# Two second layers at a time as seven products of halves, with the split input weights kept in device memory

## The chip, the cores and the metric

The kernel runs on one core of a Trainium2 chip. The metric is device time in microseconds (us) of one execution. TensorE (PE) multiplies, VectorE (DVE), ScalarE (ACT) and GpSimd (POOL) work on elements, and SyncE (SP) issues the DMAs.

## The reference, cut to what matters

```python
def reference(**kw):
    attn_out = _attn_ref(q, k, v)          # window of +-3 keys, and a branch pooled by 4; 4 x 8 heads x 576 x 64
    x = attn_out.transpose(0, 2, 1, 3).reshape(2304, 512)
    x = (sigmoid(x @ w_gate) * (x @ w_val)) @ w_out          # layer 1, 1536 hidden
    h = x @ w_in
    return (h * sigmoid(1.702 * h)) @ w_out2                 # layer 2, 2048 hidden
```

## The kernel before, in words

Attention is worked in 16 units (two heads of a batch each) and leaves x, transposed, in `att`: 512 features as 4 tiles of 128 partitions, 2304 tokens as three passes of 768. Both layers keep each pass in `att`: a layer's output takes the place of its input.

**Groups and phases.** A phase is one layer on one pass. Its hidden features are worked in groups of 256: 6 groups in layer 1 and 8 in layer 2, 42 in all, numbered k. The phases are (layer, pass) = (1,0), (1,1), (2,0), (1,2), (2,1), (2,2).

**Precision.** Every operand of a large product is a sum of a rounded part (hi) and a rest (lo), and a product is made as hi·hi + hi·lo + lo·hi. ScalarE rounds (`CAST`), GpSimd subtracts to get the lo part of weights and of x, VectorE that of the gated values g.

**Input products.** The product of x with a block of 256 hidden features is made by seven products of halves (p1 to p7, Winograd's form) of 6 matmuls of 128x384 each. A group has two blocks in layer 1 (gate and value), one in layer 2. GpSimd makes the four sums of weights that it needs, ScalarE and GpSimd split them, in each of the three phases of a layer anew from the weights as loaded (`w_raw`). VectorE combines the products (`c11`, `c12`, `c22`), ScalarE takes copies between them (`snap`), makes the gate (`sigmoid`/`gelu`) and rounds (`round_g`, L874). Three pairs of PSUM banks hold the quarters: `s_ps`, `d_ps`, `t_ps`.

**Second layer.** `second` multiplies g of a group by 256 rows of the output weights (`v_raw`, split as v_hi, v_lo) in the ordinary way through `passes` (L432): in layer 1 in 8 tiles of 6 matmuls of 384 columns, in layer 2 in 6 tiles of 6 matmuls of 512 columns. The tiles go by turns to the two banks of `o_ps`, and VectorE adds each to `att` (L1271). So TensorE's tile n waits until the tile n-2 has been added.

**Order.** Each engine's work is written out by hand, one list per engine, and an engine works its list strictly in turn; semaphores hold it where an operand isn't there. TensorE's list puts the second layer of group k between the input products of group k+1. SP's list holds the loads, each behind a wait for the buffer that it overwrites.

## Time and profile before

| | |
|---|---|
| median of 3 runs | 897.64 us (897.04 to 898.20) |
| the profiled execution: time, span | 896.92 us, 895.2 us |
| granted TensorE clock, mean | 1.00 |
| TensorE, VectorE, ScalarE, GpSimd busy | 99%, 53%, 54%, 78% |
| traffic of device memory, mean | 89 GB/s |

The span is the time between the first and the last instruction in the profile. An engine's busy time counts its operations, not its waits, and the chain that ended last says which engine's work and which waits the span is made of.

### The profile page before, as it was taken

What the parts mean: (1) busy time and instruction counts of PE and PEld (TensorE: products, weight loads), DVE (VectorE), ACT (ScalarE), POOL (GpSimd) and SP (SyncE); (2) the same over time, 40 slices, a digit from 0 to 9 for tenths busy, and PEclk for the clock granted to TensorE, in tenths of its full rate; (3) what the DMA queues carried; (4) which work ended last, traced back from release to release, by engine and by line L of the source; (5) the groups of instructions that cost most, each with busy time, mean ns of one, the idle gap of its engine ahead of it and who ended that gap; (6) DMA issues with size and microseconds to landing.
All of it is one profiled execution on the core that took longest, in us unless ns stands there. A gap on an engine that the chain in (4) does not pass through costs nothing.

```text
span 895.2 us, 17338 instructions
## 1 busy us (share of the span) xinstructions
PE 887.3 (99%) x6572; PEld 831.2 (93%) x6572; DVE 472.2 (53%) x865; ACT 483.5 (54%) x967; POOL 694.8 (78%) x551
## 2 busy tenths in 40 slices
PE   8999999999999999999999999999999999999998
PEld 6878899999999999999898899999998999989897
DVE  5767545555555455554544455555545445454545
ACT  5777755554445455545555455544645554545542
POOL 6679989998779999758787869998757887566551
PEclk9999999999999999999999999999999999999999
DMA  9776112222221222222221222422222212132111
GB/s 333 251 226 219 54 62 71 71 69 74 69 67 55 71 72 71 71 71 71 71 71 52 67 72 70 141 72 71 71 72 68 74 48 93 50 120 92 48 48 70
DMA packets 26722, 80.38 MB, mean 90 GB/s; under 512 B 2960, under 2 KB 3216, under 8 KB 26640
## 3 DMA queue, kind: packets, MB, share of 16 engines
q1 hardware_dynamic: 26640, 79.28, 27.5%
q8 instruction: 52, 0.85, 0.4%
q14 instruction: 30, 0.25, 0.1%
HBM read 74.55 MB, written 4.72 MB: 89 GB/s over the span
## 4 chain that ended last, share of the span: by engine, by line
PE 98%; DMA 1%; SPq 1%; issue 0%; DVE 0%
PE o_ps L432 39%; PE d_ps L442 7%; PE d_ps L445 7%; PE d_ps L444 7%; PE s_ps L442 6%; PE s_ps L445 6%; PE s_ps L444 6%; PE t_ps L442 3%; PE t_ps L445 3%; PE t_ps L444 3%; PE o_ps L405 1%; PE o_ps L425 1%; PE t_ps L376 1%; PE t_ps L417 1%; PE s_ps L330 1%; PE t_ps L390 1%
## 5 line engine op out<-in xcount | busy, mean ns | idle before, releaser
L1271 DVE TENSOR_TENSOR att<-o_ps,att 128x512 f32<-128x512 f32 (+1 forms) x245 | 152.4, 626 | 150.5 <-PE o_ps L432 150.5
L1518 POOL TENSOR_TENSOR w_lo<-w_sum,w_hi 128x1024 fp32r<-128x1024 f32 x60 | 144.1, 2402 | 66.0 <-ACT w_hi L782 66.0
L1513 POOL TENSOR_TENSOR w_lo<-w_raw,w_hi 128x768 fp32r<-128x768 f32 x60 | 111.0, 1849 | 44.1 <-ACT w_hi L778 44.1
L442 PE MATMUL d_ps<-xs_hi,w_hi 128*128 128x384 f32 x360 | 120.5, 335 | 0.0
L445 PE MATMUL d_ps<-xs_hi,w_lo 128*128 128x384 f32 x360 | 120.4, 335 | 0.0
L444 PE MATMUL d_ps<-xs_lo,w_hi 128*128 128x384 f32 x360 | 120.4, 334 | 0.0
L1531 POOL TENSOR_TENSOR v_lo<-v_raw,v_hi 128x1024 fp32r<-128x1024 f32 x42 | 100.7, 2398 | 20.3 <-ACT v_hi L786 20.3
L432 PE MATMUL o_ps<-v_hi,g_hi 128*128 128x512 f32 x288 | 111.9, 389 | 0.8 <-DVE att L1271 0.8
L432 PE MATMUL o_ps<-v_hi,g_lo 128*128 128x512 f32 x288 | 112.3, 390 | 0.0
L432 PE MATMUL o_ps<-v_lo,g_hi 128*128 128x512 f32 x288 | 112.3, 390 | 0.0
L1492 POOL TENSOR_TENSOR w_sum<-w_raw 128x256 f32<-128x256 f32 x120 | 88.4, 736 | 23.6 <-PE t_ps L445 20.2
L442 PE MATMUL s_ps<-xs_hi,w_hi 128*128 128x384 f32 x300 | 100.8, 336 | 0.0
L445 PE MATMUL s_ps<-xs_hi,w_lo 128*128 128x384 f32 x300 | 100.4, 335 | 0.0
L444 PE MATMUL s_ps<-xs_lo,w_hi 128*128 128x384 f32 x300 | 100.4, 335 | 0.0
L432 PE MATMUL o_ps<-g_hi,v_hi 128*128 128x384 f32 x288 | 96.3, 335 | 0.0
L432 PE MATMUL o_ps<-g_hi,v_lo 128*128 128x384 f32 x288 | 96.2, 334 | 0.0
L432 PE MATMUL o_ps<-g_lo,v_hi 128*128 128x384 f32 x288 | 96.2, 334 | 0.0
L782 ACT CAST w_hi<-w_sum 128x1024 fp32r<-128x1024 f32 x60 | 63.3, 1055 | 20.6 <-POOL w_sum L1492 20.4
L1215 DVE TENSOR_TENSOR g_lo<-t_ps,g_hi 128x384 fp32r<-128x384 f32 x90 | 49.8, 553 | 45.6 <-ACT g_hi L874 45.6
L442 PEld LDWEIGHTS d_ps<-xs_hi,w_hi 128*128 128x128 f32 x360 | 67.6, 188 | 0.6
L444 PEld LDWEIGHTS d_ps<-xs_lo,w_hi 128*128 128x128 f32 x360 | 67.6, 188 | 0.5
L445 PEld LDWEIGHTS d_ps<-xs_hi,w_lo 128*128 128x128 f32 x360 | 67.6, 188 | 0.0
(135 smaller groups left out, 1993.6 us busy)
## 6 DMA issues: line engine op xcount, KB each, us to landing
v_raw<-in_w_out_dram SPq DMA_DIRECT2D x42, 512.0 KB, 3.5
w_raw<-in_w_gate_val_dram SPq DMA_DIRECT2D x36, 512.0 KB, 3.6
w_raw<-in_w_in_dram SPq DMA_DIRECT2D x24, 512.0 KB, 3.5
vw<-in_v_win_dram SPq DMA_DIRECT2D x16, 390.0 KB, 4.9
vt<-in_v_tok_dram SPq DMA_DIRECT2D x16, 320.0 KB, 3.8
qk<-in_q_t_dram SPq DMA_DIRECT2D x16, 288.0 KB, 3.5
qk<-in_k_t_dram SPq DMA_DIRECT2D x16, 288.0 KB, 4.5
out_dram<-att SPq DMA_DIRECT2D x17, 256.0 KB, 4.5
```

What stands on the lines that cost most here:

```text
L330: mm = pe.matmul(s_ps[HK * par:HK * par + QW, h, pair * KW:(pair + 1) * KW], qu[rows, 0, PAD + at:PAD + at + QW], qu[rows, 1, at:at + KW], ...
L432: mm = pe.matmul(bank, a, b, start=(i == 0), stop=(i == len(steps) - 1))
L442: pe.matmul(bank, wh[:, w, cols], xh[:, x, c, :], start=(start and c == 0), stop=False, skip_group_check=True)
L444: pe.matmul(bank, wh[:, w, cols], xl[:, x, c, :], start=False, stop=False, skip_group_check=True)
L445: mm = pe.matmul(bank, wl[:, w, cols], xh[:, x, c, :], start=False, stop=(c == 1), skip_group_check=True)
L782: nc.scalar.copy(w_hi[b % 2][:, S1:S4 + 1, :], w_sum[b % 2][:, S1:S4 + 1, :]).then_inc(wshi_ready, 1)
L1215: vec.tensor_tensor(g_lo[k % 2][:, t, f, :], bank[LAST[k] % 2], g_hi[k % 2][:, t, f, :], ALU.subtract).then_inc(g_ready[n], 1)
L1271: vec.tensor_tensor(part, value, part, ALU.add).then_inc(y_added, 1)
L1492: return gp.tensor_tensor(w_sum[b % 2][:, name, :], a, c, op)
L1513: gp.tensor_tensor(w_lo[b % 2][:, A11:A22 + 1, :], w_raw[b % 2][:, R11:R22 + 1, :], w_hi[b % 2][:, A11:A22 + 1, :], ALU.subtract).then_inc ...
L1518: gp.tensor_tensor(w_lo[b % 2][:, S1:S4 + 1, :], w_sum[b % 2][:, S1:S4 + 1, :], w_hi[b % 2][:, S1:S4 + 1, :], ALU.subtract).then_inc(ws_re ...
L1531: gp.tensor_tensor(v_lo[k % 2][:, :, :], v_raw[k % 2][:, :, :], v_hi[k % 2][:, :, :], ALU.subtract).then_inc(v_ready, 1)
```

## The change

From the second phase on, groups go in pairs (c, d = c+1), and n = c+2 is the next pair's first. Phase 0 (groups 0 to 5) stays as it was.

1. **Second layers.** `second_pair` makes the second layers of c and d together as seven products of halves (`TILES`), two tiles each: 14 tiles of 6 matmuls of 384 columns for a pair. Its right operands are g's quarters and four sums of them, T1 to T4, which VectorE makes in PSUM (`make_t1` ...) and splits (`low_t1` ...) and ScalarE rounds (`hi_t1` ...), with copies of quarters by ScalarE (`save11`, `save12`, `save21`). Its left operands are seven pieces of the output weights of both groups (two loads into `raw`): ScalarE rounds them (`v_a12`, `v_s1`, `v_a11`, `v_s2`, `v_s4`, `v_s3`, `v_a22`), GpSimd makes four sums and seven lo parts (`split_pair`), 11 operations of 128x2x256 a pair. All 14 tiles of a pair come after the first five input products of n; p4 and p3 of n follow the tiles.
2. **Input weights.** In phase 0 the split weights of layer 1 are written to device memory (`w_split`), and those of layer 2 are split in eight separate `job`s between the pairs of phases 0 to 2 (ScalarE: `job_a`, `job_s`; GpSimd: `job_sums`, `job_lows`) and written there too. All later blocks fetch them (`fetch_12`: 786 KB and 525 KB, `fetch_3`: twice 262 KB a block); ScalarE and GpSimd don't split input weights there any more.
3. **x.** The seven split quarters and sums of x lie in a ring of 10 in place of two sets of seven. So those of the next phase are in part made early (`early_x`), and in part only when the phase's last block has read the place (`late_x`, `wait_last`), ahead of `split_pair` of the next phase's first pair in GpSimd's list.
4. **Phases** are (1,0), (1,1), (1,2), (2,0), (2,1), (2,2). The output is stored a pass at a time, the last one by tiles.

```diff
+RING = 10
...
-PHASES = [(1, 0), (1, 1), (2, 0), (1, 2), (2, 1), (2, 2)]
+OB1 = 2 * KC
+PHASES = [(1, 0), (1, 1), (1, 2), (2, 0), (2, 1), (2, 2)]
...
+TILES = ((VA12, B21, True, 0, 0), (VS1, T1, True, 1, 1), (VS4, B22, False, 0, 1), (VA11, B11, True, 0, 0),
+         (VS2, T2, False, 0, 1), (VS3, T3, False, 1, 1), (VA22, T4, False, 1, 0))
+OBP = 2 * NP
+SINCE = (8, 6, 10, 6, 4, 8, 14)
+G_OUT = {g: 2 * i + 2 for i, (v, g, start, r, t) in enumerate(TILES)}
+V_OUT = {v: 2 * i + 2 for i, (v, g, start, r, t) in enumerate(TILES)}
...
+def ring(q, x):
+    return (NP * q + x) % RING
...
+        w_split = nc.dram_tensor("w_split", (MADE + JOBS, P, 2, NP, WG), F32).ap()
...
+            def fetch_12(b):
+                if b >= NB:
+                    return
+                if b < MADE + 2:
+                    sp.wait_ge(spilled[b % 2], 16 * (MADE // 2))
+                if b == FIRST[NL1]:
+                    sp.wait_ge(job_stored, 16 * JOBS)
+                sp.wait_ge(in_done[b % 2], count(b - 2, 3))
+                sp.dma_start(w[b % 2][:, :, A11:S2 + 1, :].bitcast(F32), w_split[split_at(b), :, :, A11:S2 + 1, :]).then_inc(w_in1[b % 2], 16)
+                sp.wait_ge(in_done[b % 2], count(b - 2, 5))
+                sp.dma_start(w[b % 2][:, :, S1:S3 + 1, :].bitcast(F32), w_split[split_at(b), :, :, S1:S3 + 1, :]).then_inc(w_in2s[b % 2], 16)
...
+            def load_pair(c):
+                if c >= NG:
+                    return
+                if c == G1:
+                    sp.wait_ge(wa_ready, MADE)
+                    sp.wait_ge(wsum_ready, MADE)
+                else:
+                    sp.wait_ge(vp_ready, NP * pair(c))
+                q, lay, p, g = GROUPS[c]
+                source = w_out1 if lay == 1 else w_out2
+                for i in range(2):
+                    sp.dma_start(raw[:, i, :, :].rearrange("p a n -> p (a n)"), source[g + i]).then_inc(vp_loaded, 16)
...
+            def second_pair(c, i):
+                v_part, g_part, start, r, t = TILES[i]
+                pe.wait_ge(vp_ready, NP * pair(c) + V_LOWS[v_part])
+                if g_part in t_ready:
+                    pe.wait_ge(t_ready[g_part], strassen(c + 1))
                 else:
-                    s = o % (OB2 // 2)
-                    toks = slice(s * P, (s + 1) * P)
-                    passes(bank, [((gh[:, t, f, toks], gl[:, t, f, toks]), (vh[:, f, :], vl[:, f, :])) for f in range(FG)]
-                           ).then_inc(y_ready, 1)
+                    pe.wait_ge(g_ready[11 if g_part == B11 else 21 if g_part == B21 else 22], c + 2)
+                for j in range(2):
+                    n = y_count(c) + 2 * i + j
+                    pe.wait_ge(y_added, n - 1)
+                    cols = slice(j * P, (j + 1) * P)
+                    bank = o_ps[:, n % 2, 0:NT]
+                    for k in (c, c + 1):
+                        vh, vl = v_all[:, k % 2, 0, v_part, cols], v_all[:, k % 2, 1, v_part, cols]
+                        gh, gl = g_hi[k % 2][:, g_part, :], g_lo[k % 2][:, g_part, :]
...
+            for c in range(G1, NL1, 2):
+                if c > G1:
+                    p4(FIRST[c])
+                    p3(FIRST[c])
+                for i in range(NP):
+                    second_pair(c, i)
+            for c in range(NL1, NG - 2, 2):
+                p4(FIRST[c])
+                p3(FIRST[c])
+                head(FIRST[c + 1])
+                step(FIRST[c + 2])
+                for i in range(NP if c + 4 < NG else NP - 2):
+                    second_pair(c, i)
+            c = NG - 2
+            p4(FIRST[c])
+            p3(FIRST[c])
...
+            def round_pair_s(c, v_part, n):
+                if c >= NG:
+                    return
+                act.wait_ge(vp_summed, 4 * pair(c) + n)
+                nc.scalar.copy(v_all[:, :, 0, v_part, :], v_f[:, :, 1, v_part, :]).then_inc(vp_hi, 1)
...
+                v_a12(n)
+                hi_t4(d)
+                gelu11(n)
+                if last:
+                    round_t4(q + 1)
+                    round_b22(q + 1)
+                v_s1(n)
+                v_a11(n)
+                save11(n)
+                hi11(n)
+                gelu22(n)
+                hi22(n)
+                v_s2(n)
+                v_s4(n)
+                if n + 2 < NG:
...
+                c11(FIRST[n])
+                add(c, 0)
+                add(c, 1)
+                make_t2(d)
+                add(c, 2)
+                low_t3(d)
+                add(c, 3)
+                low_t2(d)
+                add(c, 4)
+                make_t4(d)
+                add(c, 5)
+                low_t4(d)
+                for o in range(6, 10):
+                    add(c, o)
+                if n + 2 < NG:
+                    add(c, 10)
+                low11(n)
+                if n + 2 < NG:
+                    add(c, 11)
+                c22(FIRST[n])
+                if n + 2 < NG:
+                    add(c, 12)
+                    add(c, 13)
+                low22(n)
...
+            def split_pair(c):
+                steps = 4 * pair(c)
+                pair_low(c, VA12, raw[:, :, V12, :])
+                pool.wait_ge(vp_loaded, 32 * pair(c) + 32)
+                pool.wait_ge(y_ready, v_free(c, VS1))
+                pair_sum(VS1, raw[:, :, V21, :], raw[:, :, V22, :], ALU.add)
+                pair_low(c, VA11, raw[:, :, V11, :])
+                pool.wait_ge(y_ready, v_free(c, VS2))
+                pool.wait_ge(vp_summed, steps + 1)
+                pair_sum(VS2, v_f[:, :, 1, VS1, :], raw[:, :, V11, :], ALU.subtract)
+                pool.wait_ge(vp_summed, steps + 2)
+                pair_sum(VS4, raw[:, :, V12, :], v_f[:, :, 1, VS2, :], ALU.subtract)
+                pair_low(c, VS1, v_f[:, :, 1, VS1, :])
+                pool.wait_ge(vp_summed, steps + 3)
+                pair_low(c, VS2, v_f[:, :, 1, VS2, :])
+                pair_low(c, VS4, v_f[:, :, 1, VS4, :])
+                pool.wait_ge(y_ready, v_free(c, VS3))
+                pair_sum(VS3, raw[:, :, V11, :], raw[:, :, V21, :], ALU.subtract)
+                pair_low(c, VS3, v_f[:, :, 1, VS3, :])
+                pair_low(c, VA22, raw[:, :, V22, :])
...
+            def late_x(q):
+                next_t1_t3_sums(q)
+                next_t1(q)
+                next_t3(q)
+                next_t4_sums(q)
+                next_t4(q)
+                next_b22(q)
```

**ScalarE around the tiles of a layer 2 pair.** In the list of before, in the last phase (w_ is an input weight, v_ an output weight, s_ps a pair of quarters of the products):

```order
L848 ACTIVATE s_ps<-s_ps 128x384 [waits c11_ready]
L874 CAST g_hi0_100<-s_ps 128x384 [waits y_ready,gated11]
L843 COPY snap2_69<-s_ps 128x384 [waits c22_ready,in_done0]
L778 CAST w_hi1_53<-w_raw1_65 128x768 [waits in_done1,w_loaded1]
L848 ACTIVATE s_ps<-s_ps 128x384 [waits c22_ready]
L874 CAST g_hi0_100<-s_ps 128x384 [waits y_ready,gated22]
L786 CAST v_hi0_58<-v_raw0_62 128x1024 [waits v_loaded0]
L782 CAST w_hi1_53<-w_sum1_57 128x1024 [waits wsum_ready]
L848 ACTIVATE s_ps<-s_ps 128x384 [waits in_done0]
```

and after the change in the same phase, ahead of a pair c's last tiles (raw and v_f are an output weight and its sum; `g_f0` is a saved quarter):

```order
L1028 CAST v_74<-raw_76 128x2x256 [waits y_ready,vp_loaded]
L1131 COPY g_f0_112<-s_ps 128x384 [waits y_ready,gated11]
L1150 CAST g_hi0_110<-s_ps 128x384 [waits y_ready,gated11]
L1109 ACTIVATE s_ps<-s_ps 128x384 [waits c22_ready]
L1150 CAST g_hi0_110<-s_ps 128x384 [waits y_ready,gated22]
L1035 CAST v_74<-v_f_75 128x2x256 [waits vp_summed] x3
L1109 ACTIVATE s_ps<-s_ps 128x384 [waits in_done0]
L1138 COPY g_f0_112<-s_ps 128x384 [waits y_ready,gated21]
L1150 CAST g_hi0_110<-s_ps 128x384 [waits y_ready,gated21]
```

Before, the output weights were cast in one piece that waits for its load alone (L786), and the cast of the input weights' sums (L782) stood ahead of the activation of quarter 21, which waits for `in_done0`. Now three casts of sums of output weights (L1035), each of which waits for a sum of GpSimd (`vp_summed`), stand in that place.

**GpSimd in the same phase.** Before, one group's work (four sums and two lo parts of input weights, the lo part of output weights):

```order
L1492 TENSOR_TENSOR w_sum0_56<-w_raw0_64 128x256 [waits in_done0,w_loaded0]
L1492 TENSOR_TENSOR w_sum0_56<-w_sum0_56,w_raw0_64 128x256 [waits wsum_step]
L1492 TENSOR_TENSOR w_sum0_56<-w_raw0_64 128x256
L1492 TENSOR_TENSOR w_sum0_56<-w_raw0_64,w_sum0_56 128x256 [waits wsum_step]
L1513 TENSOR_TENSOR w_lo0_54<-w_raw0_64,w_hi0_52 128x768 [waits wahi_ready]
L1518 TENSOR_TENSOR w_lo0_54<-w_sum0_56,w_hi0_52 128x1024 [waits wshi_ready]
L1531 TENSOR_TENSOR v_lo1_61<-v_raw1_63,v_hi1_59 128x1024 [waits vhi_ready]
```

and now a pair's (the first rows of `split_pair`, without the lo part of the first piece that stands ahead of them):

```order
L2036 TENSOR_TENSOR v_f_75<-raw_76 128x2x256 [waits y_ready,vp_loaded]
L2040 TENSOR_TENSOR v_74<-raw_76,v_74 128x2x256 [waits vp_hi]
L2036 TENSOR_TENSOR v_f_75<-v_f_75,raw_76 128x2x256 [waits vp_summed,y_ready]
L2036 TENSOR_TENSOR v_f_75<-raw_76,v_f_75 128x2x256 [waits vp_summed]
L2040 TENSOR_TENSOR v_74<-v_f_75,v_74 128x2x256 [waits vp_hi]
L2040 TENSOR_TENSOR v_74<-v_f_75,v_74 128x2x256 [waits vp_hi,vp_summed]
L2040 TENSOR_TENSOR v_74<-v_f_75,v_74 128x2x256 [waits vp_hi]
L2036 TENSOR_TENSOR v_f_75<-raw_76 128x2x256 [waits y_ready]
```

Each lo part waits for ScalarE's cast (`vp_hi`), and the last sum stands behind four lo parts that wait so.

**VectorE during the tiles.** Before, around the first tiles of a group:

```order
L1215 TENSOR_TENSOR g_lo1_103<-t_ps,g_hi1_101 128x384 [waits ghi11_ready]
L1271 TENSOR_TENSOR att_70<-o_ps,att_70 128x512 [waits y_added,y_ready]
L1202 TENSOR_TENSOR t_ps<-snap2_69,t_ps 128x384 [waits g11_ready,u3_ready]
L1271 TENSOR_TENSOR att_70<-o_ps,att_70 128x512 [waits y_added,y_ready] x2
L1215 TENSOR_TENSOR g_lo1_103<-t_ps,g_hi1_101 128x384 [waits ghi22_ready]
L1271 TENSOR_TENSOR att_70<-o_ps,att_70 128x512 [waits y_added,y_ready] x3
L1206 TENSOR_TENSOR t_ps<-snap1_68,t_ps 128x384 [waits in_done1]
```

and now during a pair's 14 tiles:

```order
L1713 TENSOR_TENSOR att_80<-o_ps,att_80 128x384 [waits y_added,y_ready] x2
L1658 TENSOR_TENSOR t_ps<-t_ps,g_f1_115 128x384 [waits thi_ready4,t_ready3]
L1713 TENSOR_TENSOR att_80<-o_ps,att_80 128x384 [waits y_added,y_ready]
L1669 TENSOR_TENSOR g_lo1_114<-t_ps,g_hi1_113 128x384 [waits thi_ready4]
L1713 TENSOR_TENSOR att_80<-o_ps,att_80 128x384 [waits y_added,y_ready]
L1669 TENSOR_TENSOR g_lo1_114<-t_ps,g_hi1_113 128x384 [waits thi_ready2]
L1713 TENSOR_TENSOR att_80<-o_ps,att_80 128x384 [waits y_added,y_ready]
L1665 TENSOR_TENSOR t_ps<-g_f1_115,t_ps 128x384 [waits ghi21_ready,t_ready2]
L1713 TENSOR_TENSOR att_80<-o_ps,att_80 128x384 [waits y_added,y_ready]
L1669 TENSOR_TENSOR g_lo1_114<-t_ps,g_hi1_113 128x384 [waits thi_ready5]
L1713 TENSOR_TENSOR att_80<-o_ps,att_80 128x384 [waits y_added,y_ready] x5
```

The sums T2 and T4 of the group d and three lo parts now stand between the adds (L1713), one other operation to an add, up to the sixth.

## Rows read from the trace of the kernel before

**Rows 1.** Page, part 1 (busy time, share, instructions) and 2 (clock in 40 slices).

```profile
span 895.2 us, 17338 instructions
...
PE 887.3 (99%) x6572; PEld 831.2 (93%) x6572; DVE 472.2 (53%) x865; ACT 483.5 (54%) x967; POOL 694.8 (78%) x551
...
PEclk9999999999999999999999999999999999999999
```

**Rows 2.** Page, part 4: shares of the chain that ended last.

```profile
PE 98%; DMA 1%; SPq 1%; issue 0%; DVE 0%
```

**Rows 3.** Chain in order of time: start, us, engine, tile, line, count.

```profile
242.51 2.08 PE o_ps L432 x12
...
265.39 2.08 PE o_ps L432 x12
...
385.03 4.16 PE o_ps L432 x24
...
842.97 8.20 PE o_ps L432 x36
858.47 8.20 PE o_ps L432 x36
```

**Rows 4.** GpSimd by line and shape: count, busy us, mean ns, idle before.

```profile
L1518 POOL TENSOR_TENSOR w_lo<-w_sum,w_hi 128x1024 fp32r<-128x1024 f32 x60 | 144.1, 2402 | 66.0 <-ACT w_hi L782 66.0
L1513 POOL TENSOR_TENSOR w_lo<-w_raw,w_hi 128x768 fp32r<-128x768 f32 x60 | 111.0, 1849 | 44.1 <-ACT w_hi L778 44.1
...
L1492 POOL TENSOR_TENSOR w_sum<-w_raw 128x256 f32<-128x256 f32 x120 | 88.4, 736 | 23.6 <-PE t_ps L445 20.2 <-PE d_ps L445 2.4
...
L1536 POOL TENSOR_TENSOR xs_lo<-xs_sum,xs_hi 128x768 fp32r<-128x768 f32 x24 | 43.7, 1842 | 0.0
...
L1474 POOL TENSOR_TENSOR half_sum<-qk 128x576 f32<-128x576 f32 x16 | 18.3, 1145 | 1.1 <-DMA qk<-in_k_t_dram 1.1
```

**Rows 5.** ScalarE by line and shape, the same columns.

```profile
L778 ACT CAST w_hi<-w_raw 128x768 fp32r<-128x768 f32 x60 | 50.4, 840 | 0.0
...
L874 ACT CAST g_hi<-t_ps 128x384 fp32r<-128x384 f32 x90 | 43.6, 484 | 1.3 <-DVE t_ps L1211 0.2
```

**Rows 6.** Timeline of 386 to 388.6 us: start, us, engine, operation.

```profile
386.10 0.56 DVE L1271 TENSOR_TENSOR att<-o_ps,att 128x384 f32<-128x384 f32 x1
...
386.78 0.19 PEld L432 LDWEIGHTS o_ps<-g_hi,v_hi 128*128 128x128 f32 x1
386.95 0.33 PE L432 MATMUL o_ps<-g_hi,v_hi 128*128 128x384 f32 x1
...
387.14 0.56 DVE L1271 TENSOR_TENSOR att<-o_ps,att 128x384 f32<-128x384 f32 x1 [0.48 <-PE o_ps L432]
...
387.62 0.55 DVE L1215 TENSOR_TENSOR g_lo<-d_ps,g_hi 128x384 fp32r<-128x384 f32 x1
...
388.18 0.56 DVE L1271 TENSOR_TENSOR att<-o_ps,att 128x384 f32<-128x384 f32 x1
```

**Rows 7.** Timeline of 776.6 to 780.8 us, ScalarE to VectorE.

```profile
776.82 0.48 ACT L831 COPY snap<-d_ps 128x384 f32<-128x384 f32 x1 [1.09 <-PE d_ps L445]
...
777.19 0.49 ACT L848 ACTIVATE d_ps<-d_ps 128x384 f32<-128x384 f32 x1
...
777.71 0.48 ACT L874 CAST g_hi<-d_ps 128x384 fp32r<-128x384 f32 x1
...
779.79 0.48 ACT L874 CAST g_hi<-t_ps 128x384 fp32r<-128x384 f32 x1
...
780.30 0.56 DVE L1215 TENSOR_TENSOR g_lo<-t_ps,g_hi 128x384 fp32r<-128x384 f32 x1 [1.05 <-ACT g_hi L874]
```

**Rows 8.** Timeline of 506 to 507.5 us, TensorE behind an add.

```profile
506.47 0.50 PE L432 MATMUL o_ps<-v_hi,g_hi 128*128 128x512 f32 x1 [0.77 <-DVE att L1271]
```

**Rows 9.** Page, part 2 (GB/s in 40 slices) and part 6 (DMA issues).

```profile
GB/s 333 251 226 219 54 62 71 71 69 74 69 67 55 71 72 71 71 71 71 71 71 52 67 72 70 141 72 71 71 72 68 74 48 93 50 120 92 48 48 70
...
v_raw<-in_w_out_dram SPq DMA_DIRECT2D x42, 512.0 KB, 3.5
```

More of the change, by code:

```diff
@@ new lines, in last_pair @@
+            def last_pair(c):
+                d = c + 1
+                gelu21(c)
+                save21(c)
+                hi21(c)
+                gelu12(c)
+                snap_p1(FIRST[d])
+                save12(c)
+                gelu11(d)
+                snap_u2(FIRST[d])
+                hi_t1(c)
+                save11(d)
+                hi11(d)
+                snap_u3(FIRST[d])
+                gelu22(d)
+                hi_t3(c)
+                v_s3(c)
+                gelu12(d)
+                save12(d)
+                hi_t2(c)
+                gelu21(d)
+                save21(d)
+                hi21(d)
+                hi22(d)
+                v_a22(c)
+                hi_t1(d)
+                hi_t4(c)
+                hi_t3(d)
+                hi_t2(d)
+                hi_t4(d)
@@ new lines, in last_pair @@
+            def last_pair(c):
+                d = c + 1
+                c12(FIRST[c])
+                low21(c)
+                c11(FIRST[d])
+                make_t1(c)
+                make_t3(c)
+                low_t1(c)
+                low11(d)
+                c22(FIRST[d])
+                add(c - 2, 10)
+                add(c - 2, 11)
+                c12(FIRST[d])
+                make_t2(c)
+                low_t3(c)
+                low_t2(c)
+                make_t1(d)
+                low21(d)
+                add(c - 2, 12)
+                low22(d)
+                add(c - 2, 13)
+                make_t3(d)
+                low_t1(d)
+                make_t4(c)
+                add(c, 0)
+                low_t4(c)
+                add(c, 1)
+                make_t2(d)
+                low_t3(d)
+                add(c, 2)
+                low_t2(d)
+                add(c, 3)
+                make_t4(d)
+                add(c, 4)
+                low_t4(d)
+                for o in range(5, OBP):
+                    add(c, o)
```

1405 lines of the change are left out of this document (850 added, 555 removed).

## The prediction

> **What bounds the kernel now.** I read the page first. TensorE is busy 99% of a span of 895.2 us [rows 1] and makes up 98% of the chain that ended last [rows 2], with a granted clock of 9 tenths or more in every slice [rows 1]. So TensorE alone bounds it, and a change helps only by taking matmuls away and keeping TensorE fed. The pieces of the chain price a matmul: 24 of 384 columns in 4.16 us, so 0.173 us each and 1.04 for a tile or product of six; 36 of 512 columns in 8.20, so 0.228 each [rows 3]. A layer 2 group passes in 858.47 - 842.97 = 15.50 us, two in 31.0; a layer 1 group in 265.39 - 242.51 = 22.88 [rows 3].
>
> **Matmuls removed.** A layer 1 pair had 2 x 8 x 6 = 96 matmuls of 384 columns in its second layers and has 84: 12 x 0.173 = 2.08 us, in 6 pairs 12.5. A layer 2 pair had 72 of 512 columns (16.40) and has 84 of 384 (14.56): 1.84 us, in 12 pairs 22.1. Together -34.6. All else on TensorE (products, attention) stays. If nothing waited, the span would be 860.6. The profiled time is 1.7 above its span, and the median of the runs 0.7 above the profiled time.
>
> **Prices of what feeds TensorE.** GpSimd: 736 ns for 256 elements, 1849 for 768, 2402 for 1024 [rows 4]; on that line 512 elements (128x2x256) take D = 1.29 us. One row lies off it, 576 elements in 1.145 [rows 4], by which D would be 1.02. These are the two ends. I take 1.29, since the off row is of attention and the others have the kinds of operands that the new ones have. The Trainium skill, GPSIMD Engine Reference, section 3.1, gives about 2.6 cycles per element for a two-input operation; worked out, as an estimate, that adds 1.11 us plus a fixed part for 512 elements, which is nearer to the first end, and the rows of 256 to 1024 agree in slope. ScalarE: 484 ns for 384 and 840 for 768 [rows 5], so 0.60 for 512; operations that don't depend on each other start 0.37 apart, dependent ones 0.52 [rows 7]. A VectorE add or lo part of 384 takes 0.56, and one add with one other operation 0.48 + 0.56 = 1.04, just one tile [rows 6]. From ScalarE to VectorE 0.03 [rows 7]. An add starts 0.19 after the next tile's first matmul, and the tile after that loads its weights 0.12 after the add has ended [rows 6]: between the tiles there is next to no slack, and a VectorE operation late by more than 0.1 during the tiles stops TensorE. That such a stop happens shows the matmul at 506.47, 0.77 idle behind an add [rows 8]. A load of 512 KB lands after 3.5 us, and the fastest slice moved 333 GB/s [rows 9].
>
> **An inner layer 2 pair** (8 of them). S is the start of its tile 0; tile k should start at S + 1.04k, the 14 end at 14.56, p4 and p3 of n at 16.64, p1, p2 of its partner at 18.72, and then p6 needs ScalarE's snap. No wait would make a pair 29.12.
> (a) The output weights of the next pair. SP's list has their load behind `fetch_12`, whose second part waits for p7, the product just before S. It is issued at S + 0.7 to 1.0 behind 525 KB and the rest of 786 KB, and 1 MB more at 333 GB/s lands near S + 7.0 (bounds: 4.5, by the 3.5 of [rows 9] if nothing else was on its way, and 8). `v_a12` runs from 7.0 to 7.6 and holds `hi_t4` to 8.0 and VectorE's `low_t4` to 8.6. Add 6 stands behind that, and tile 8 starts at 9.4 and not at 8.32: +1.04 (bounds 0 and 1.1).
> (b) GpSimd then works nine operations in turn until the sum VS3 is there: lo, sum, lo, sum, sum, three los, sum. 7.6 + 9 x 1.29 = 19.2, and `v_s3` ends at 19.8. In ScalarE's list `gelu21`, `save21`, `hi21`, `gelu12` and the snap of p1 stand behind it; so the snap ends at 21.9, where 18.7 was wanted. TensorE's p6 waits 3.2. By D = 1.02 it would be 0.8, by a landing at 4.5 also 0.7, by both nothing. To be free of it `v_s3` would have to start by S + 15.9.
> (c) `low_t4` of c stands behind `c12` of d on VectorE, and p5 of n waits for it: +0.4 (bounds 0, 0.6).
> Sum 4.65 a pair, so 33.8 us, 2.8 more than the 31.0 of before. 8 x 4.65 = +37.2.
>
> **The ends of phases in layer 2** (c = 24 and 32). `late_x` splits the next phase's x in GpSimd's list, in operations of 1.84 us [rows 4], ahead of `split_pair`. Before the tiles, counted from the end of p7 of d: `snap_u3` and `v_a22` until 1.3, lo VA22 2.6, sum T1 4.4, sum T3 6.3, lo T1 8.1, lo T3 9.9. p7 of n needs that last one, and would start at 6.2: +3.7. Then (a) again: +1.0. `round_t4` stands on ScalarE behind `v_a12` (S + 7.6), `hi_t4` and `gelu11` and ends at 9.7; lo T4 ends at 11.6, lo B22 13.5, lo VA12 14.8, sum VS1 16.1; `v_s1`, `v_a11`, `save11` and `hi11` end at 18.0. VectorE has `low11` ahead of add 11, so tile 13 starts at 19.2 where 14.6 was left to it: +4.6. The rest of `split_pair` puts the snap of p1 late by another 4.6. Together 14.0 each: +28.0. For the pair c = 38, whose list is its own, I put 4, and 0.8 for the last stores: +4.8.
>
> **Layer 1.** A pair has four blocks of products and not two, 14.6 us of TensorE more to hide in, so (b) shrinks. An inner pair has 1.8 for `v_s3` ahead of the activations of n, 0.3 for `low_t1`, which holds add 0 and so tile 2, and 0.3 for p2 of d's value block: 2.45. c = 12: 3.0. In c = 8 and 14 ScalarE and GpSimd also stand at jobs whose load SP issues behind the store of the job before, 3.8 more: 6.2 each. c = 10 and 16 have a phase's end, as above, with less of it late: 11.7 and 12.6. c = 6, the first: its seven casts of output weights stand in ScalarE's list among the snaps and in chain with GpSimd, which has `late_x` before them: p7 and p4 of block 15 wait 2.6 and 8.9, then 2.45: 14. Between phase 0 and 1 p6, p5 and p4 of the first block wait for x pieces that are split late (1.4 + 1.4 + 3.0): 5.8. Together 14 + 6.2 + 11.7 + 3.0 + 6.2 + 12.6 + 5.8 = +59.5. These are my least certain terms: bounds half and 1.2 times.
>
> **Of no price.** Traffic rises: a layer 2 pair fetches 2 x 1.84 MB and 1.05, so 4.7 MB in 29 to 34 us, 140 to 162 GB/s against 333 that a slice shows [rows 9]. GpSimd's sum falls from 78%, ScalarE's stays; no engine's busy time comes near TensorE's. What costs is order, not work.
>
> **Sum.** 895.2 - 34.6 + 37.2 + 28.0 + 4.8 + 59.5 = 990.1; with 1.7 to 2.4 around it 992. Where waits fall together, one late engine finds the next one late too and part is counted twice; I take 990.
>
> **Rivals.**
> - *Half the waits.* D is 1.02 or the load lands early, so (b) is 0 to 0.8, and the boundary terms, which are made of GpSimd's time, shrink by a third to a half. Stalls of 55 to 90: 917 to 952. For it: one row with 1.145; against it: four rows on the other line.
> - *Faster.* The lists are met in time: `v_s3` starts before S + 15.9 everywhere, and `late_x` is covered. Then only (a), (c) and single boundaries are left, 3 to 20 us, and the time is 864 to 880. For it: the mean busy shares leave room, GpSimd has 14.2 us to do in 29. It decides if the waits are under 34.6 in all. Against it: the chain of nine operations behind a load that can't be issued before S.
> - *The clock falls.* Before, TensorE never idles, and its clock stays at the higher level (2.4 GHz). Waits of 5 to 9 us at a phase's end could bring it to 1.2 GHz for a while. Matmuls take twice as long at it, so if each of 4 to 10 such waits is followed by 10 us at that level, 5 us are lost each time: 1010 to 1040. The Trainium skill, TensorE: Matmul & The Clock Gate, section "Why this matters for your kernels", warns that gaps between bursts of matmuls lower the clock; the trace of before has no gap by which to weigh it.
>
> **How the numbers follow.** The forecast (slower by waits that stand in the lists) 0.70, its own range 955 to 1008; half the waits 0.13; clock 0.05; faster 0.12. Leaving out faster, and most of the clock case, the range is 917 to 1012. A measurement of this kernel can tell about 0.2% from no change. Faster by more than that 0.12, within 0.02 (waits of just 33 to 36 us), slower 0.86.
>
> **What would show it.** In the profile after: 84 matmuls of 384 columns to a pair at 0.173 us, TensorE's busy sum near 853; its share of the span 86 to 88%; p6 of d waiting for a snap by ScalarE some 3 us a pair, ScalarE idle at the casts of v_f for GpSimd; GpSimd's 128x2x256 at 1.29 us; a landing of `raw` 6 us after its issue; the longest gaps at c = 6, 10, 16, 24 and 32. I would be wrong if D is near 1.0, if the load of `raw` lands before S + 5, or if ScalarE runs through its list without idling at `v_s3`.

## The result, and the profile after

The changed kernel takes 1044.06 us (median of 4 runs, 1041.15 to 1050.79) against 897.92 of before (897.04 to 898.66): ratio 1.164, 95% interval 1.158 to 1.170. It is slower by 146 us. The forecast was 990 with a range of 917 to 1012, so the direction was right and the size was not.

From the page (span, busy time of each engine, the granted clock in 40 slices, the chain that ended last; to be read against [rows 1] and [rows 2]):

```profile
span 1042.8 us, 18514 instructions
...
PE 915.2 (88%) x6638; PEld 871.8 (84%) x6638; DVE 585.1 (56%) x1128; ACT 528.3 (51%) x1191; POOL 594.9 (57%) x483
...
PEclk9999999998989999999999999898999988898899
...
PE 52%; POOL 19%; issue 10%; ACT 8%; DMA 6%; DVE 4%; SPq 1%; ACTq 0%; DVEq 0%; POOLq 0%
```

TensorE fell from 99% to 88% of the span, and from 98% to 52% of the chain: now it waits. Two more things stand there. TensorE's busy time is 915.2 us, where 887.3 less the 34.6 of matmuls taken away would be 853, so each matmul took longer on the average. And the granted clock shows eights where it had nines; its mean over the span is 0.949. What TensorE waited for (engine, line, releaser; us in total, times, longest):

```profile
PE d_ps L632 <- ACT snap L1072: 44.2, 17, 5.8
PE o_ps L776 <- DVE att L1713: 29.8, 14, 4.1
PE s_ps L632 <- ACT snap L1078: 9.4, 2, 4.8
PE d_ps L632 <- ACT snap L1084: 8.5, 1, 8.5
PE d_ps L632 <- issue: 7.8, 3, 3.4
```

L1072, L1078 and L1084 are ScalarE's three snaps, L1713 is VectorE's add.

**One pair, read in time.** In the pair whose tile 0 starts at 916.6, the two loads of the next output weights are issued here (start, us):

```profile
917.36 1.07 SPq L390 DMA_DIRECT2D raw<-in_w_out_dram  x2
```

and ScalarE's first cast of them (v_a12) stands idle until they have landed:

```profile
925.24 0.62 ACT L1028 CAST v<-raw 128x512 fp32r<-128x512 f32 x1 [4.81 <-DMA raw<-in_w_out_dram]
```

That is 8.6 us after tile 0. VectorE's `low_t4` is late by it, so a tile waits 2.3 us. Then, after the pair's tiles, GpSimd's sum VS3, ScalarE's list and TensorE's p6:

```profile
938.67 1.28 POOL L2036 TENSOR_TENSOR v_f<-raw 128x512 f32<-128x512 f32 x1
...
939.33 0.34 PE L634 MATMUL t_ps<-xs_hi,w 128*128 128x384 f32 x1
939.98 0.62 ACT L1035 CAST v<-v_f 128x512 fp32r<-128x512 f32 x1 [3.44 <-POOL v_f L2036]
940.50 0.47 ACT L1109 ACTIVATE s_ps<-s_ps 128x384 f32<-128x384 f32 x1
...
941.01 0.48 ACT L1138 COPY g_f<-s_ps 128x384 f32<-128x384 f32 x1
941.38 0.48 ACT L1150 CAST g_hi<-s_ps 128x384 fp32r<-128x384 f32 x1
941.75 0.50 ACT L1109 ACTIVATE d_ps<-d_ps 128x384 f32<-128x384 f32 x1
...
942.16 0.49 ACT L1072 COPY snap<-d_ps 128x384 f32<-128x384 f32 x1
...
942.71 0.69 PE L632 MATMUL d_ps<-xs_hi,w 128*128 128x384 f32 x1 [3.04 <-ACT snap L1072]
```

VS3's sum runs from 938.67. ScalarE takes it at 939.98, and `gelu21`, `save21`, `hi21`, `gelu12` and the snap follow one another; TensorE, which could have gone on at 939.5, starts p6 at 942.71. This is the place of step (b) of the forecast, and its size, 3 us. But both ends of that wait are some 4 us later than forecast: the snap ends 26.0 us after tile 0 and not 21.9, and TensorE wants it at 22.9 and not at 18.7. The rows just behind the wait show something else; look at the starts:

```profile
943.19 0.53 PE L633 MATMUL d_ps<-xs_lo,w 128*128 128x384 f32 x1
943.51 0.53 PE L634 MATMUL d_ps<-xs_hi,w 128*128 128x384 f32 x1
943.83 0.53 PE L632 MATMUL d_ps<-xs_hi,w 128*128 128x384 f32 x1
```

These starts are 0.32 us apart, where [rows 3] has 0.173. It goes on so until 948.9, for 18 matmuls, and that costs 2.9 us. 384 columns in 0.32 us are 1.2 GHz, the lower of the clock's two levels, and the granted clock of this stretch (942.7 to 948.9) is 0.50. GpSimd's operations on 512 elements are no part of it; they have the price that was forecast, D = 1.28:

```profile
L2040 POOL TENSOR_TENSOR v<-v_f,v 128x512 fp32r<-128x512 f32 x72 | 91.1, 1280 | 21.2 <-ACT v L1035 21.2
...
L2036 POOL TENSOR_TENSOR v_f<-raw 128x512 f32<-128x512 f32 x36 | 46.2, 1282 | 5.5 <-PE o_ps L778 5.5
```

**The account.** I add up, over the timeline, the distances between the starts of neighbouring 384-column matmuls: what a wait adds (some 0.2 us more than the idle time in brackets), and what matmuls add that are more than 0.21 apart without a wait, from the first tile of a second layer on. Before: 0 and 0.5 us (its one wait, of [rows 8], is at a matmul of 512 columns). After: 128.4 us of waits and 50.6 us of slow matmuls. 860.6 (the span without waits, from the forecast) + 128.4 + 50.6 = 1039.6; the span is 1042.8, and 2.8 of the rest lie before the first tile, which came at 125.5 before and at 128.3 here (124.6 to 128.3 in the traces of this case, with the same attention). About 4 of the 50.6 us are not the clock's: the matmul behind the first one after a wait starts 0.25 to 0.28 later also where all that follow are 0.173 apart. The forecast had 129.5 us of waits and nothing for the clock.

### The profile page after: what moved, and what is told of

Its sections match the earlier page's. It is cut to its first block, busy times and chain, and to the rows that moved or that the text cites. A ratio compares the mean times of both kernels' runs of the same rounds, so it can differ in the third digit from the quotient of the medians.

```text
span 1042.8 us, 18514 instructions
## 1 busy us (share of the span) xinstructions
PE 915.2 (88%) x6638; PEld 871.8 (84%) x6638; DVE 585.1 (56%) x1128; ACT 528.3 (51%) x1191; POOL 594.9 (57%) x483
## 4 chain that ended last, share of the span: by engine, by line
PE 52%; POOL 19%; issue 10%; ACT 8%; DMA 6%; DVE 4%; SPq 1%; ACTq 0%; DVEq 0%; POOLq 0%
POOL v L2040 7%; PE o_ps L776 5%; POOL v_f L2036 5%; PE o_ps L778 5%; PE o_ps L777 5%; PE d_ps L632 4%; POOL xs_lo L2067 4%; DMA raw<-in_w_out_dram 4%; PE d_ps L633 4%; PE d_ps L634 4%; PE o_ps L623 4%; PE s_ps L632 3%; PE s_ps L634 3%; PE s_ps L633 3%; DMA job_raw<-in_w_in_dram 2%
## 5 line engine op out<-in xcount | busy, mean ns | idle before, releaser
L776 PE MATMUL o_ps<-g_hi,v 128*128 128x384 f32 x504 | 177.4, 352 | 29.8 <-DVE att L1713 29.8
L632 PE MATMUL d_ps<-xs_hi,w 128*128 128x384 f32 x360 | 128.6, 357 | 68.8 <-ACT snap L1072 44.2
L778 PE MATMUL o_ps<-g_hi,v 128*128 128x384 f32 x504 | 175.5, 348 | 0.0
L777 PE MATMUL o_ps<-g_lo,v 128*128 128x384 f32 x504 | 175.4, 348 | 0.0
L1713 DVE TENSOR_TENSOR att<-o_ps,att 128x384 f32<-128x384 f32 x212 | 117.2, 556 | 73.8 <-PE o_ps L778 72.2
L776 PEld LDWEIGHTS o_ps<-g_hi,v 128*128 128x128 f32 x504 | 100.1, 199 | 34.6 <-POOL v L2040 18.7
L634 PE MATMUL d_ps<-xs_hi,w 128*128 128x384 f32 x360 | 125.2, 348 | 0.0
L633 PE MATMUL d_ps<-xs_lo,w 128*128 128x384 f32 x360 | 125.1, 348 | 0.0
L632 PE MATMUL s_ps<-xs_hi,w 128*128 128x384 f32 x300 | 106.0, 353 | 19.6 <-ACT snap L1078 9.4
L634 PE MATMUL s_ps<-xs_hi,w 128*128 128x384 f32 x300 | 104.3, 348 | 0.0
L633 PE MATMUL s_ps<-xs_lo,w 128*128 128x384 f32 x300 | 103.9, 346 | 0.0
L2040 POOL TENSOR_TENSOR v<-v_f,v 128x512 fp32r<-128x512 f32 x72 | 91.1, 1280 | 21.2 <-ACT v L1035 21.2
L777 PEld LDWEIGHTS o_ps<-g_lo,v 128*128 128x128 f32 x504 | 100.1, 199 | 0.0
L778 PEld LDWEIGHTS o_ps<-g_hi,v 128*128 128x128 f32 x504 | 99.5, 197 | 0.0
L1035 ACT CAST v<-v_f 128x512 fp32r<-128x512 f32 x72 | 43.2, 620 | 107.8 <-POOL v_f L2036 107.4
L632 PEld LDWEIGHTS s_ps<-xs_hi,w 128*128 128x128 f32 x300 | 59.0, 197 | 24.8 <-ACT snap L1078 11.3
```

Of the source, the lines that this page charges most:

```text
L632: pe.matmul(bank, wh[:, cols], xh[:, c, :], start=(start and c == 0), stop=False, skip_group_check=True)
L633: pe.matmul(bank, wh[:, cols], xl[:, c, :], start=False, stop=False, skip_group_check=True)
L634: mm = pe.matmul(bank, wl[:, cols], xh[:, c, :], start=False, stop=(c == 1), skip_group_check=True)
L776: pe.matmul(bank, vh, gh, start=(start and k == c), stop=False, skip_group_check=True)
L777: pe.matmul(bank, vh, gl, start=False, stop=False, skip_group_check=True)
L778: mm = pe.matmul(bank, vl, gh, start=False, stop=(k == c + 1), skip_group_check=True)
```

## The experiments

The same account was taken of each run (times: medians, each ratio to runs of the kernel before from the same session; waits and slow matmuls: of the profiled execution; in e3 without the 20.8 us of the matmuls that were put in).

| run | us | ratio to before, 95% | waits | slow |
|---|---|---|---|---|
| the change | 1044.1 | 1.158 to 1.170 | 128.4 | 50.6 |
| e1_early | 1015.1 | 1.129 to 1.133 | 106.7 | 45.5 |
| e2_order | 989.4 | 1.099 to 1.106 | 85.3 | 43.0 |
| e3_fill | 1029.4 | 1.144 to 1.148 | 106.9 | 38.1 |
| e4_both | 961.4 | 1.068 to 1.075 | 65.0 | 31.1 |
| e5_ends | 937.6 | 1.044 to 1.049 | 55.3 | 17.3 |
| e6_first_jobs | 947.4 | 1.055 to 1.059 | 56.3 | 27.9 |
| e7_all | 931.2 | 1.036 to 1.041 | 50.0 | 17.4 |
| e8_tuned | 899.3 | 1.001 to 1.004 | 24.3 | 10.4 |
| e9_pause (of before) | 935.0 | 1.040 to 1.044 | 29.7 | 7.3 |
| e10_last | 899.7 | 1.001 to 1.004 | 24.8 | 12.4 |
| e11_start | 904.4 | 1.004 to 1.009 | 27.4 | 12.1 |
| e12_final | 895.8 | 0.997 to 0.999 | 18.7 | 11.6 |

**e1_early: the load alone.**

```diff
                 for b in (FIRST[c + 1], FIRST[c + 2]):
                     fetch_3(b + 1)
+                    if b == FIRST[c + 2]:
+                        load_pair(c + 2)
                     fetch_12(b + 2)
-                load_pair(c + 2)
```

> The changed kernel with one edit: in layer 2 the load of the next pair's output weights is issued before the fetch of split input weights that waits for p7, about 3 us ahead of the tiles. In the changed kernel it lands 8.6 us after tile 0, and inner layer 2 pairs lose 0.9 to 3.3 us between tiles 7 and 11, with 1.6 us of matmuls at the lower clock behind most of them. Theory A (the last sum VS3 is late because GpSimd's lo part of VS2 waits for ScalarE's cast behind the activation of quarter 22): the tile waits go, the wait of p6 for the snap stays at 3 us, and the time falls by 20 to 27 us, to about 1020. Theory B, the prediction's (GpSimd's nine operations count from the landing): p6's wait falls under 1 us too, and the time falls to 965 to 985. Theory C (the loads cost nothing): within 3 us of 1044.

Measured 1015.1, 29 us less. (In the two profiled executions 3.4 us of it lie before the first product of layer 1, which the edit doesn't touch; waits and slow matmuls give 26.8, the upper end of what Theory A expected.) TensorE's waits for snaps and for adds:

```profile
PE d_ps L633 <- ACT snap L1073: 41.9, 17, 5.8
PE o_ps L777 <- DVE att L1714: 13.2, 5, 4.1
```

The inner pairs' waits for adds are gone (29.8 to 13.2; the five left are of phase ends and the program's end), but p6's stay: 41.9 where 44.2 was, 3.0 us at each inner pair. Theory A holds. The forecast's arithmetic for (b), nine operations counted from the landing, doesn't: by it p6 would have waited 1 us or less. In the pair whose tile 0 starts at 896.8 the load has landed by 901.6, and still:

```profile
910.08 0.55 DVE L1596 TENSOR_TENSOR s_ps<-snap,d_ps 128x384 f32<-128x384 f32 x1
910.66 0.47 ACT L1110 ACTIVATE s_ps<-s_ps 128x384 f32<-128x384 f32 x1 [2.25 <-DVE s_ps L1596]
911.54 1.14 ACT L1036 CAST v<-v_f 128x512 fp32r<-128x512 f32 x2
912.31 2.54 POOL L2041 TENSOR_TENSOR v<-v_f,v 128x512 fp32r<-128x512 f32 x2 [0.86 <-ACT v L1036]
914.81 1.27 POOL L2037 TENSOR_TENSOR v_f<-raw 128x512 f32<-128x512 f32 x1
```

GpSimd's lo part of VS2 waits for ScalarE's cast (L1036), which stands behind the activation of quarter 22 and `hi22`; that activation waits for VectorE's `c22` (L1596), and `c22` comes only after add 11. So the chain up to VS3's sum (the last row) hangs on the tiles too, and not on the landing alone.

**e2_order: VS3's cast behind the snap.**

```diff
                 v_s2(n)
                 v_s4(n)
-                if n + 2 < NG:
-                    v_s3(n)
...
                 snap_p1(FIRST[d])
+                v_s3(c)
                 save12(c)
```

(in layer 1 the same, behind the snap of the pair's second block).

> The changed kernel with one edit: ScalarE's cast of VS3 stands behind the snap of p1 of the next block and no longer ahead of the four operations before that snap, in both layers. Theory A (this place in the list makes p6 wait 3.0 to 3.2 us a layer 2 pair and 1.6 a layer 1 pair, and each wait of 3 us is followed by 5 to 6 us of matmuls at the lower clock): about 11 x 3.1 + 4 x 1.6 = 40 us of waiting go and 15 to 20 us of slow matmuls, so 985 to 992. Rival (no clock cost hangs on these waits): 1004. Rival (the snap is late for other reasons, or the next snap is late in its place): 1025 or above.

Measured 989.4. The big group of waits, L1072 with 44.2, is down to 1.6. Two of those that are left:

```profile
PE o_ps L776 <- DVE att L1712: 30.9, 14, 4.1
...
PE d_ps L632 <- ACT snap L1078: 4.7, 5, 2.0
```

43 us of waits went and 7.6 of slow matmuls, where 40 and 15 to 20 were expected. So the place that Theory A names is shown, but the clock's cost doesn't hang on the waits one by one, and that the time lies within 985 to 992 is in part luck: 2.5 us of the gain lie before the first product of layer 1. (The medians lie 55 us apart, the two profiled spans 53.)

**e3_fill: TensorE kept at work through the wait.**

```diff
                 p1(b)
                 p2(b)
+                for i in range(12):
+                    pe.matmul(o_ps[:, y % 2, 0:NT], wh[:, 0:P], xh[:, 0, :], start=True, stop=True, ...)
                 p6(b)
```

> The changed kernel with 12 extra matmuls of 384 columns (2.1 us at 0.173) on 11 places in layer 2, between p2 and p6 of the pair's second block, where TensorE waits 3 us for a snap. They write to a bank that the next tile overwrites; the output is not changed. Theory A (idle TensorE is what lowers the clock): the 3 us wait is filled, the matmuls behind it stay at 0.173 us instead of 0.32, and with 132 matmuls more the time falls by 12 to 25 us, to 1019 to 1032. Rival (the clock falls for the mean load or for another reason): no gain, and the granted clock at these places stays down. Rival (the extra matmuls just add): 1044 to 1067.

Measured 1029.4, 15 us less. (There are ten such places and 120 matmuls more, not 11 and 132. In the kernel the loop stands in a helper of its own, behind a wait for the last add of that bank.) In the timeline of TensorE, the twelve and what follows them:

```profile
966.60 2.25 PE L727 MATMUL o_ps<-xs_hi,w 128*128 128x384 f32 x12
969.80 0.44 PE L632 MATMUL d_ps<-xs_hi,w 128*128 128x384 f32 x1 [0.95 <-ACT snap L1081]
970.08 0.34 PE L633 MATMUL d_ps<-xs_lo,w 128*128 128x384 f32 x1
970.25 0.34 PE L634 MATMUL d_ps<-xs_hi,w 128*128 128x384 f32 x1
```

The wait is now 0.95 us, and the starts behind it are 0.17 apart; the granted clock there is 1.00. In the changed kernel 6 of these ten waits had slow matmuls behind them, 12.5 us in the ten places together; in this run none has, and 1.1 is left of the 12.5. This is the one run that separates the two costs: the snap comes no sooner (the last matmul of p2 and the first of p6 start 3.1 to 3.6 us apart), TensorE has more to do, and 12.5 us of slow matmuls are gone over the whole span. Of the rest of the 15 us, 1.9 lie before the first product of layer 1.

**e4_both: e1 and e2.**

> Both edits, early load and VS3's cast behind the snap. If the two waits are independent and each brings its clock loss, the gains of the two add: -22 and -55, so 960 to 975. What is left then are the waits at phase ends, at the first pair and at the jobs of layer 1, some 60 us with 20 us of lower clock. If the second wait only hid the first, the sum is less than the better one by over 15 us.

Measured 961.4: the gains (29 and 55) add to 84, 83 came. An inner layer 2 pair passes in 30.0 us, less than the 31.0 of before.

**e5_ends: the ends of phases**, on top of e4 (its core, layer 2; `last` is a phase's last pair, `first` its first):

```diff
                 snap_p1(FIRST[d])
-                v_s3(c)
+                if first:
+                    v_s2(c)
+                    v_s4(c)
+                else:
+                    v_s3(c)
+                    v_a22(c)
...
-                v_s1(n)
-                v_a11(n)
+                if not last:
+                    v_s1(n)
+                    v_a11(n)
                 save11(n)
                 hi11(n)
```

> On top of both edits, the lists at the ends of phases are put in another order: ScalarE rounds T2 and T1 of the next phase earlier, the casts of VA22 stand before GpSimd's next sums, and where a phase ends the casts of the output weights' sums stand behind what the tiles and snaps need. In the run with both edits TensorE waits 35 us at these places (3.6 twice, 3.1, 4.2, and about 10 twice) and has 16 us of matmuls at the lower clock behind them. Theory A (these waits come from the order of the lists, each brings its clock loss, and nothing else is late there): 961 - 48 = 913, between 908 and 925. Rival (GpSimd simply has too much to do at the ends, 13 us of x and 14 of weights): the waits move to other places and the time stays above 935.

Measured 937.6, half of the gain expected and above the 935 of the rival. But the rival's reason, GpSimd's load, is not what the trace shows. The waits at the ends shrank (a phase's end in layer 2 had 7 to 10 us and has 4 to 5), and new ones came from the moved casts: VA22's cast, put early in all pairs, brought 0.8 at each inner pair, and the casts of a phase's first layer 1 pair held a snap for 3.8. e8 takes most of both away by order alone.

**e6_first_jobs: the first pair and the jobs**, on top of e4.

```diff
+                if c == G1:
+                    v_a12(c)
                 hi22(c)
...
-                if c == G1:
-                    v_a12(c)
-                    v_s1(c)
-                    v_a11(c)
...
-                    if c in (G1 + 2, G1 + 8) and b == FIRST[c + 1]:
+                    if c in (G1 + 2, G1 + 8) and b == LAST[c + 1]:
...
-                if c in (G1, G1 + 6):
-                    store_job(2 if c == G1 else 5)
-                    load_job(3 if c == G1 else 6)
+                    if c in (G1, G1 + 6) and b == LAST[c + 1]:
+                        store_job(2 if c == G1 else 5)
+                        load_job(3 if c == G1 else 6)
```

> On top of both edits, layer 1 alone: the casts of the first pair's output weights are spread over its input products, the loads and stores of the jobs are issued one block earlier, and the second job of a pair is cast during the tiles. In the run with both edits TensorE waits 2.2 and 7.6 us in the first pair and 4.7 and 5.8 for snaps behind the jobs, with 8.5 us of lower clock. Theory A (waits of the list's order, and a load that is issued late behind a store): 961 - 28 = 933, between 929 and 940. Rival (the store of a job, 1.8 MB, needs too long whatever the order): the job waits stay, 945 or above.

Measured 947.4. The first pair's waits fell from 9.8 to 2.1 us. At the jobs the rival's time came (945 or above), but not by its reason. The edit did not issue all jobs earlier, as was expected of it: the first two changed lines issue the second job of a pair a block later. Its load landed 4 us into the tiles, and the tiles waited 3.5 where a snap had waited 4.7. The load of the first job, issued a block earlier, cured the snap's wait; with the two lines taken back and the casts moved, e8 waits no more than 1.1 us at the jobs. So the order does matter.

**e7_all: e5 and e6.**

> All edits together. If all of the loss is waits of the lists' order and the clock behind them, the gains add: 961 - 48 - 28 = 885, within 878 to 895, and so below the kernel before (897). The products of halves then give back 12 of the 34.6 us that they save on TensorE. If something else takes time in the changed kernel (slower matmuls, traffic), it stays above 897.

Measured 931.2, above the range. The gains were 23.8 and 14.0 apart and are 30.2 together. Nothing else takes time, though: 860.6 + 50.0 of waits + 17.4 of slow matmuls are 928.0 in a span of 929.6. What is left are waits, some of them brought by the moves.

**e8_tuned: the lists once more**, each move at a wait that e7's trace named (two of eight are shown).

```diff
                 snap_u3(FIRST[d])
+                hi_t2(c)
...
                 snap_p1(FIRST[n])
                 gelu22(d)
-                hi_t2(c)
...
                 make_t4(c)
-                c12(FIRST[d])
                 low_t4(c)
+                c12(FIRST[d])
```

> The kernel with all edits, its lists put in order once more at the waits that are left in it: the job's store again at the earlier block, its casts behind the snap that they held, the casts VS2 to VA22 of a phase's first layer 1 pair behind the snaps, VA22 of inner layer 2 pairs back in its old place, T2 and T4 of group c rounded and split before the next block's snap and combination, T3 of the next x earlier. The kernel with all edits has 50 us of waits and 17 of lower clock. Theory A (order again): about 32 of them go, 899, between 892 and 912. Rival (GpSimd and ScalarE now are what limits layer 1): above 920.

Measured 899.3, on the forecast. Waits 24.3, slow matmuls 10.4: together 34.7, just what the seven products save. (The profiled execution took 896.9, the shortest of six.)

**e9_pause: waits put into the kernel before.**

```diff
                 p2(n)
+                if k in PAUSES:
+                    pe.wait_ge(paused, 16 * PAUSES.index(k) + 16)
                 p6(n)
```

> The kernel before, with TensorE made to wait: in 8 groups of the first two layer 2 phases p6 waits for a copy of 512 KB that is issued after p1, in 3 groups of the last phase for one of 32 KB; nothing else is changed. By the landing times of loads TensorE should stand still about 3.4 us at each of the 8 places and 1.4 us at each of the 3, 31 us in all. Theory A (standing still some 3 us lowers TensorE's clock, and that costs 1.6 to 2.9 us more behind each wait): 897 + 31 + 13 to 23 = 941 to 951, with matmuls 0.32 apart behind the 8 waits and 0.17 behind the 3. Rival (the lower clock in the changed kernel is due to its traffic or its mean load, not to the waits): 928, and the matmuls stay 0.17 apart.

Measured 935.0, 37.3 more than before: 29.7 of waits and 6.8 of slow matmuls. That is between the 941 to 951 of the theory and the 928 of the rival. The longest wait, on TensorE's timeline:

```profile
672.77 0.69 PE L450 MATMUL d_ps<-xs_hi,w_hi 128*128 128x384 f32 x1 [4.08 <-DMA spare<-in_w_in_dram]
673.26 0.52 PE L452 MATMUL d_ps<-xs_lo,w_hi 128*128 128x384 f32 x1
673.58 0.52 PE L453 MATMUL d_ps<-xs_hi,w_lo 128*128 128x384 f32 x1
```

The granted clock from there to 678.6 is 0.51. One of the short waits:

```profile
876.01 0.45 PE L450 MATMUL d_ps<-xs_hi,w_hi 128*128 128x384 f32 x1 [0.99 <-DMA spare<-in_w_in_dram]
876.29 0.34 PE L452 MATMUL d_ps<-xs_lo,w_hi 128*128 128x384 f32 x1
876.47 0.33 PE L453 MATMUL d_ps<-xs_hi,w_lo 128*128 128x384 f32 x1
```

So waiting alone, without the change and its traffic, slows the matmuls behind it. But it did so behind 3 of the 8 longer waits (4.2, 4.2 and 2.8 us), not behind the other five (2.8 to 3.1), and behind none of the three short ones (1.2 to 1.3). In the changed kernel it is 19 of 24 waits of over 2.2 us, and at two of the other five the slow matmuls come 1.7 us later, behind a second wait of 0.6. So a single wait of 3 us is a chance of the loss, not the loss.

**e10_last: four more moves on e8.**

> The kernel tuned last, with four more moves at waits that its trace shows: T1 of the second phase is rounded behind the snap and split before the sum T3 is made (1.8 + 1.2 us of waits at 239 to 242), the adds of the last two tiles of the pair before the last stand ahead of T1 and of the lo part of quarter 21 (1.8 us at 876), and the casts of two jobs stand behind one more snap (twice 1.1). Theory (all that is left are waits of order): about 4.5 us go, 895, between 892 and 898, just below the kernel before. Rival (they turn up one step later): 899.

Measured 899.7. The jobs' waits of 1.1 us went, but between phase 0 and 1 waits of 2.2 and 3.2 us took the place of 1.8, 1.2 and 1.4, and at the end a wait of 1.7 stands where 1.8 was. The time is that of e8, and the rival was right.

**e11_start: the first pair of a phase.**

> The kernel tuned before the last one (899.3), so without the last one's moves at phase 0 and at the end, which brought new waits there, but with its move of the two jobs' casts (both waits of 1.1 us went in that trace), and with one more: in the first pair of each layer 2 phase the casts VS2 and VS4 stand behind both snaps, VS3 and VA22 behind the tiles' start. That pair waits 0.8 for a snap, 0.8 for a lo part and 0.6 for a snap, with up to 1.0 of lower clock, three times. Theory: twice 0.9 and three times 2.3 to 3 us go: 891, between 888 and 895, below the kernel before. Rival (GpSimd's lo parts of these pieces are then late for tile 8 or 10 of the pair): 896 to 900, with waits on o_ps.

Measured 904.4, above what theory and rival expected. The first pairs passed in 29.7 us instead of 32.0, as meant, and their followers waited. SP's loads for the follower were issued here:

```profile
671.25 0.81 SPq L390 DMA_DIRECT2D raw<-in_w_out_dram  x2
```

and landed here, on ScalarE's timeline:

```profile
678.26 0.62 ACT L1029 CAST v<-raw 128x512 fp32r<-128x512 f32 x1 [6.92 <-DMA raw<-in_w_out_dram]
```

In e8 they were issued at 663.3. The load waits for the lo part of VA22, which I had put later: cause (a) of the first experiment once more, made by hand.

**e12_final: e8 with the jobs' move, and two small ones that leave VA22 alone.**

```diff
-                    v_s4(c)
...
                 snap_u2(FIRST[d])
+                if first:
+                    v_s4(c)
...
+                hi_t2(c)
                 if first:
                     v_s3(c)
                 if not last:
                     v_a22(c)
-                hi_t2(c)
```

> The kernel of 899.3 with the move of the two jobs' casts and with two small moves in the first pair of each layer 2 phase, which leave VS3 and VA22 early: VS4's cast behind the second snap, and the rounding of T2 of group c ahead of VS3's cast. In the run before, VA22 late meant that the load of the next output weights, which waits for its lo part, was issued 8 us later (671.3 and not 663.3), and a tile waited 2.6 to 4.7 us. Theory: that wait does not come, and twice 0.9 and three times 1.5 to 3 us go: 892, between 889 and 896, below the kernel before (898). Rival (a new wait again): 898 or more.

Measured 895.8 (12 runs, 893.95 to 897.35) against 897.35 of before (17 runs): ratio 0.998, 0.997 to 0.999. The page's head:

```profile
span 892.5 us, 18514 instructions
...
PE 868.8 (97%) x6638; PEld 831.0 (93%) x6638; DVE 585.5 (66%) x1128; ACT 526.8 (59%) x1191; POOL 597.5 (67%) x483
...
PEclk9999999999999999999999999999999999999999
```

It is the only one below the kernel before, by 1.5 us of the 34.6 that the change takes off TensorE, and just inside the 889 to 896 expected.

## Why the prediction was wrong

- **Matmuls removed, -34.6: right.** The account closes with it in all variants of the changed kernel, from 1044 to 896 us, to within 3.2 us.
- **Prices: right.** D was 1.28 against 1.29 taken; casts 0.62 against 0.60.
- **The sum of the waits, 129.5 against 128.4: right in part by luck.** The inner layer 2 pairs were 9.4 us longer than forecast, the ends of phases in layer 2 and layer 1 together 11.0 shorter, and the last two pairs 0.6 longer.
- **An inner layer 2 pair, 4.65: right in place, too small: 4.7 to 6.8, mean 5.8.** (a) was 0.9 to 3.3, mean 2.2, and not 1.0; in the pair shown the load landed at S + 8.6 and not 7.0. (c) was 0.3. (b) measured 3.2 to 3.4 in all eight, as forecast, but not by the path forecast: GpSimd doesn't work its nine operations in turn. In the pair shown they take 14.1 us and not 11.6, since it waits 2.6 for ScalarE's casts between them. That, and the later landing, puts the snap 4 us later; TensorE comes 4 us later too, by the wait of the tile and the slow matmuls behind it. What I said of (b)'s bounds, 0.7 for an early landing, was false (e1). And with a snap at S + 21.9 whatever the tiles do, (a) ought not to have been added to (b) at all; that the two do add (e4) comes of the part of the chain that hangs on the tiles.
- **Ends of phases in layer 2, 14.0 each: measured 11.3 and 10.5.** The first: 4.7 before the tiles, 3.7 at tile 13, 2.9 at the snap.
- **Layer 1:** c = 6 12.6 (14 forecast), c = 8 and 14 6.7 and 6.5 (6.2), c = 10 10.1 (11.7), c = 12 1.8 (3.0), c = 16 10.4 (12.6), phase 0 to 1 5.8 (5.8). The jobs' part was caused as I said, by a load behind a store (10.3 us to landing); with that load issued a block earlier the snap's wait of 4.7 is gone (e6).
- **The clock: the step that failed.** The sum has no term for it. It stood among the rivals as "waits of 5 to 9 us at a phase's end could bring it to 1.2 GHz for a while", at 4 to 10 places, with a chance of 0.05. Waits of 2.3 to 3.4 us, of which I myself forecast one in each pair, did it as well: 50.6 us of slow matmuls in all. With that the forecast's 990 is 1041, outside its range of 917 to 1012; the measured time is 1044. The trace of before has no gap over 0.8 us to weigh the rival by, and I took the absence of evidence for a small chance. The sign that I named, TensorE at 86 to 88% of the span, came true (88%), but with 915 us of busy time and not 853. e3 shows the cause (same snap, TensorE busy, clock kept), e9 shows it without the change.

What stays open: why one wait of 2.8 us is followed by slow matmuls and another of 3.1 is not. Between single waits of e9 I found no difference in the rows, and the share in the changed kernel, where waits follow one another in 15 us, is higher; that the distance is the reason is not shown. I tried no kernel that changes the distance between waits alone.

## What to carry to other kernels

When work is taken off an engine that is busy 99% of the time, the sum of all waits that the new order brings decides, and each wait costs more than its length: in this kernel, where waits of 2 to 4 us come often, it was some 40% on top (50.6 on 128.4), in e9, with few of them, 23% (6.8 on 29.7). A wait that can't be removed can be filled with work on TensorE; 12 matmuls of no use in each of ten waits took 12.5 us of slow matmuls away. In a list that is worked strictly in turn, a cast that waits for another engine belongs behind everything that the bounding engine waits for: moving one cast in ScalarE's lists gained 55 us, and moving one load of SP's list 29. But only as far as nothing else waits for that cast: put later still, VA22 held back the next load (e11).
